# Two expert stages: the second stage's first group taken from a constant address, ahead of the tables

## The reference, cut to what matters

```python
X = fft(fft(x, axis=1), axis=2).real                 # (4, 2496, 256) -> x of 9984 rows x 256
# stage 1: each token to one expert of 8, at most 1248 tokens each
out[mask] = relu(x[mask] @ w1[e]) @ w2[e]            # w1: 256 x 1024, w2: 1024 x 256
# stage 2: each token to its best expert, no limit
e_idx = argmax(x @ w_gate)
gate_w = softmax(x @ w_gate)[e_idx];  eom = sigmoid(x @ w_output_gate)[e_idx]
out[mask] = gate_w * eom * (relu(x[mask] @ w1b[e]) @ w2b[e])
```

## Time and profile before

| | us |
|---|---|
| median of 3 runs | 1352.18 (1351.89 to 1353.84) |
| the profiled execution | 1355.83 |
| its span in the trace | 1354.1 |
| PE busy | 1277.1 (94%) |
| DVE busy | 761.8 (56%) |
| POOL busy | 520.2 (38%) |
| ACT busy | 324.8 (24%) |
| chain that ended last | PE 74%, DVE 11%, issue 2% |

### The profile page before, as it was taken

One profiled execution on the slowest core, in us unless ns is written; L12 is line 12 of the kernel. 1 busy time (PEld: TensorE's weight loads), 2 busy tenths in 40 slices (PEclk: granted clock), 3 DMA queues, 4 the chain that ended last, 5 costly groups with the idle time before them and its releaser, 6 DMA issues.

```text
span 1354.1 us, 30708 instructions
## 1 busy us (share of the span) xinstructions
PE 1277.1 (94%) x10392; PEld 1175.9 (87%) x10393; DVE 761.8 (56%) x2029; ACT 324.8 (24%) x787; POOL 520.2 (38%) x531
## 2 busy tenths in 40 slices
PE   8998999579999999999999997999999999999996
PEld 5666888558879888889999996999999999999996
DVE  6935888878585678775443544433333334333332
ACT  1013010122322323333232331222222222222221
POOL 0000011226465656555657541612443252544411
PEclk9999555579999999999999998999999999999998
DMA  7717241022212121212222221221232121232110
GB/s 322 269 62 264 91 141 64 1 76 70 83 54 87 58 83 59 75 63 87 61 84 77 68 86 43 87 68 40 78 107 74 43 90 52 77 107 75 47 39 20
DMA packets 63129, 115.98 MB, mean 86 GB/s; under 512 B 7736, under 2 KB 45377, under 8 KB 62912
## 3 DMA queue, kind: packets, MB, share of 16 engines
q1 hardware_dynamic: 39264, 72.16, 15.5%
q0 software_dynamic: 11808, 31.03, 7.0%
q10 hardware_dynamic: 11968, 11.63, 3.2%
HBM read 81.64 MB, written 34.45 MB: 86 GB/s over the span
## 4 chain that ended last, share of the span: by engine, by line
PE 74%; DVE 11%; issue 2%; DMA 1%; ACT 1%; POOL 0%; ACTq 0%; DVEq 0%; POOLq 0%; SPq 0%
PE bank L1105 22%; PE bank L1107 22%; PE bank L1106 21%; PE bank L986 3%; PE bank L969 3%; DVE hot_r L1784 2%; PE bank L1254 1%; PE bank L1117 1%; DVE hot_q L1785 1%; DVE hot_q L1783 1%; DVE hT_low L1954 1%; DVE arena L1663 1%; DVE xT_low L1947 0%; DVE arena L1728 0%; DVE arena L1657 0%
## 5 line engine op out<-in xcount | busy, mean ns | idle before, releaser
L1105 PE MATMUL bank<-weights_high,hT_high 128*128 (+1 forms) x1328 | 388.6, 293 | 0.0
L1107 PE MATMUL bank<-weights_high,hT_low 128*128 (+1 forms) x1328 | 378.4, 285 | 0.0
L1106 PE MATMUL bank<-weights_low,hT_high 128*128 (+1 forms) x1328 | 377.2, 284 | 0.0
L1105 PE MATMUL bank<-xT_high,weights_high 128*128 128x256 f32 (+2 forms) x1072 | 335.2, 313 | 9.2 <-DVE hT_low L1954 3.7
L1107 PE MATMUL bank<-xT_high,weights_low 128*128 128x256 f32 (+2 forms) x1072 | 331.1, 309 | 0.0
L1106 PE MATMUL bank<-xT_low,weights_high 128*128 128x256 f32 (+2 forms) x1072 | 330.4, 308 | 0.0
L1106 PEld LDWEIGHTS bank<-weights_low,hT_high 128*128 128x128 f32 x1328 | 250.4, 189 | 0.0
L1105 PEld LDWEIGHTS bank<-weights_high,hT_high 128*128 128x128 f32 x1328 | 250.2, 188 | 0.1
L1107 PEld LDWEIGHTS bank<-weights_high,hT_low 128*128 128x128 f32 x1328 | 250.2, 188 | 0.0
L1105 PEld LDWEIGHTS bank<-xT_high,weights_high 128*128 128x128 f32 x1072 | 204.6, 191 | 24.5 <-DVE hT_low L1954 7.8
L1107 PEld LDWEIGHTS bank<-xT_high,weights_low 128*128 128x128 f32 x1072 | 203.9, 190 | 11.3
(11 more groups left out here) (264 smaller groups left out, 1404.4 us busy)
## 6 DMA issues: line engine op xcount, KB each, us to landing
arena<-middle ACTq DMA_DIRECT2D x44, 258.0 KB
spectrum<-arena SPq DMA_DIRECT2D x39, 256.0 KB, 2.2
arena<-in_w2a_t SPq DMA_DIRECT2D x8, 1024.0 KB, 4.8
raw<-in_w1a SPq DMA_DIRECT2D x8, 1024.0 KB
raw<-in_w2a SPq DMA_DIRECT2D x8, 1024.0 KB
raw<-in_w1b SPq DMA_DIRECT2D x8, 1024.0 KB
raw<-in_w2b SPq DMA_DIRECT2D x8, 1024.0 KB
arena<-in_x SPq DMA_DIRECT2D x4, 768.0 KB, 4.4
```

The costliest lines, as they stand in the source:

```text
L1105: pe.matmul(out_, a[0], b[0], start=start, stop=False)
L1106: pe.matmul(out_, a[0], b[1], start=False, stop=False)
L1107: return pe.matmul(out_, a[1], b[0], start=False, stop=stop)
```

## The change

Expert 0 always gets at least one group (`cnt` of expert 0 is at least 1), so the first group is always rows 0 to 255 of `middle` with expert 0's weights, and needs no table. SP loads it (`first_rows`) once the last expert's first group has been scattered; `late_i` says whether expert 0 had fewer than 256 rows by then, and in that case SP waits for all scatters. TensorE turns and multiplies group 0 ahead of its wait for `m2.row`. The jump over the redo block stands ahead of group 0 on all engines; on DVE it moves ahead of `list_tables`, which follows the differences of group 0. The 24 spins go; nine stand ahead of the last `places`, and the four behind the jump follow the transposes. ACT issues the load of group 1 between the third and the fourth quarter's cast of group 0. TensorE's order for group 0 is hidden(0), read of `last_i`, result(0) tile 0, turn(1), result(0) tile 1, hidden(1); the loop starts at 1 instead of 0.

```diff
@@ SP, behind the loads of the second stage's first two weights
+            def first_rows(done):
+                sp.dma_start(xg_all, middle[0:W2, :].rearrange("(j p) r -> p j r", p=P)).then_inc(done, 16)
+
+            sp.wait_ge(m1.place, E * NG - NG + 1)
+            sp.sem_inc(s_hold, 1)
+            late = sp.value_load(late_i[0:1, 0:1], min_val=0, max_val=1)
+            sp.wait_ge(m1.sent[0], 16 * TILES[0] * E)
+            for gi in range(1, NG):
+                sp.wait_ge(m1.sent[gi], late * (16 * TILES[gi]) + 16 * TILES[gi] * (E - 1))
+            first_rows(m2.got)
             sp.wait_ge(s_flag, 1)
@@ PE, places and expert
+                    if first_count:
+                        pe.matmul(bank[7][:, w * E:w * E + E], ones_b[:], kinds_up[gi][:, :, w], start=True, stop=True)
                     pe.matmul(to, tri_b[:], ...)
...
-                        places(e, gi)
+                        elif fast:
+                            pe.wait_ge(m1.h, E * NG * FCH + 3)
+                            pe.wait_ge(m1.split, (E + 1) * SPLITS)
+                            spin(SPIN_KINDS)
+                        places(e, gi, fast and last and gi == 0)
@@ PE, behind the first stage
             list_counts()
-            pe.wait_ge(m1.h, E * NG * FCH + 3)
-            pe.wait_ge(m1.split, (E + 1) * SPLITS)
-            spin(SPIN_TABLES)
             pe.wait_ge(s_flag, 1)
...
-            spin(SPIN_BRANCH)
...
-            def result2(i):
+            def result2(i, slot=None, tiles=range(GP)):
...
+            x_turn2(0)
+            spin(SPIN_BRANCH)
+            pe.wait_ge(m2.xT, 2 * GP)
+            hidden_from(0, E % 2)
             pe.wait_ge(m2.row, 1)
             pe.sem_inc(s_hold, 1)
             last = pe.value_load(last_i[0:1, 0:1], min_val=MIN2 - 1, max_val=G2 - 1)
-            x_turn2(0)
-            hidden2(0)
-            with pe.Fori(0, last) as i:
+            result2(0, E % 2, [0])
+            x_turn2(1)
+            result2(0, E % 2, [1])
+            hidden2(1)
+            with pe.Fori(1, last) as i:
@@ ACT
-            def h_out2(i):
+            def h_out2(i, first=0, stop=HB):
...
+            x_out2(0)
+            h_out2(0, 0, HB - 1)
             for gi in range(NG):
                 act.wait_ge(m1.sent[gi], 16 * TILES[gi] * E)
+            act.wait_ge(m2.gt, GP)
             act.wait_ge(m2.row, 1)
             act.sem_inc(s_hold, 1)
+            load2(1)
             last = act.value_load(last_i[0:1, 0:1], min_val=MIN2 - 1, max_val=G2 - 1)
-            load2(0)
-            x_out2(0)
-            act.wait_ge(m2.gt, GP)
-            act.sem_inc(s_hold, 1)
-            load2(1)
-            h_out2(0)
+            h_out2(0, HB - 1)
@@ DVE
+                    if first_count:
+                        dve.tensor_scalar(late_i[:], bank[7][0:1, w * E:w * E + 1], float(W2), None, ALU.is_lt)
...
+                link(dve.tensor_scalar(cnt[:, 0:1], cnt[:, 0:1], 1.0, None, ALU.max))
...
-            list_tables(link, 1, m2.row)
             dve.wait_ge(s_flag, 1)
...
-            dve.sem_inc(m2.xT, GP)
-            dve.sem_inc(m2.h, HB)
-            dve.sem_inc(m2.y, GP)
+            x_out2(0)
+            list_tables(m2.row)
+            gate_out2(0)
+            h_out2(0)
             dve.wait_ge(m2.row, 1)
             dve.sem_inc(s_hold, 1)
             last = dve.value_load(last_i[0:1, 0:1], min_val=MIN2 - 1, max_val=G2 - 1)
-            x_out2(0)
-            h_out2(0)
             wants()
             x_out2(1)
+            gate_out2(1)
             empties()
             y_out2(0)
             h_out2(1)
```

More of the change, by code:

```diff
@@ L80 @@
 MIN2 = N // W2
-SPIN_START, SPIN_LISTS, SPIN_TURN, SPIN_TABLES, SPIN_BRANCH = 24, 12, 2, 24, 4
+SPIN_START, SPIN_LISTS, SPIN_TURN, SPIN_KINDS, SPIN_BRANCH = 24, 12, 2, 9, 4
 HB = 4
@@ L381, in build_program @@
         end_f, run_f, want_f, same_f = (sb(n, [P, G2 + 1]) for n in ("end_f", "run_f", "want_f", "same_f"))
+        late_i = sb("late_i", [1, 1], I32)
         expert_i, want_i, last_i = sb("expert_i", [1, G2], I32), sb("want_i", [1, G2 + 1], I32), sb("last_i", [1, 1], I32)
@@ L663, in _ @@
                 sp.wait_ge(again.raw, (E + 1) * 32 + 32)
+                for gi in range(NG):
+                    sp.wait_ge(again.sent[gi], 16 * TILES[gi] * E)
+                sp.wait_ge(m2.got, 16)
+                first_rows(again.raw)
+                sp.wait_ge(again.raw, (E + 1) * 32 + 48)
                 sp.sem_inc(s_hold, 1)
@@ L1153, in result, with places @@
                     mm.then_inc(m.y_ps, 1)
-                def places(e, gi):
+                def places(e, gi, first_count=False):
                     w = TILES[gi]
@@ L1206, in list_counts @@
             def list_counts():
-                pe.matmul(bank[0][:, 0:E], ones_b[:], kinds_up[NG - 1][:, :, TILES[NG - 1]], start=True,
+                pe.matmul(bank[5][:, 0:E], ones_b[:], kinds_up[NG - 1][:, :, TILES[NG - 1]], start=True,
                           stop=True).then_inc(s_list, 1)
             list_counts()
-            pe.wait_ge(m1.h, E * NG * FCH + 3)
-            pe.wait_ge(m1.split, (E + 1) * SPLITS)
-            spin(SPIN_TABLES)
             pe.wait_ge(s_flag, 1)
@@ L1244, in _ @@
                 pe.wait_ge(again.tables, 1)
+                pe.wait_ge(again.raw, (E + 1) * 32 + 48)
                 pe.sem_inc(s_hold, 1)
-            spin(SPIN_BRANCH)
             def x_turn2(i):
@@ L1267, in hidden2, with hidden_from @@
                     with pe.If(slot == s):
[L1268 to L1276, removed]
-            def result2(i):
-                slot = group_expert(i) & 1
-                for j in range(GP):
+                        hidden_from(i, s)
+            def hidden_from(i, s):
+                for q in range(HB):
+                    pe.wait_ge(m2.h, i * HB + (q + 1))
+                    for n, f in enumerate(range(q * FCH // HB, (q + 1) * FCH // HB)):
+                        for c in range(DCH):
+                            o = first_at(c, f)
+                            mm = three(bank[H_BANKS[q]][:, n * W2:(n + 1) * W2],
+                                       [t[:, o:o + P] for t in w_split[s]],
+                                       [t[:, c, 0:W2] for t in xT_split], c == 0, c == DCH - 1)
+                    mm.then_inc(m2.h_ps, 1)
+            def result2(i, slot=None, tiles=range(GP)):
+                if slot is None:
+                    slot = group_expert(i) & 1
+                for j in tiles:
                     pe.wait_ge(m2.y, i * GP + (j + 1))
@@ L1444, in x_out2 @@
                              bank[j][:, 0:D].rearrange("p (c n) -> p c n", c=DCH)).then_inc(m2.xT_high, 1)
-            def h_out2(i):
-                for q in range(HB):
+            def h_out2(i, first=0, stop=HB):
+                for q in range(first, stop):
                     act.wait_ge(m2.h_ps, i * HB + (q + 1))
@@ L1994, in routed, with placed @@
                         dve.tensor_copy(kinds_in[(gi + 1) % NG][:, :, 0], kup[:, :, w])
-                def placed(e, gi):
+                def placed(e, gi, first_count=False):
                     k0, w = FIRSTS[gi], TILES[gi]
@@ L2043, in expert @@
                             gated(e, gi)
-                        placed(e, gi)
+                        placed(e, gi, fast and last and gi == 0)
                 return x_out, h_out, expert
@@ L2051, in _ @@
             dve.sem_inc(m1.h, 3)
+            dve.sem_inc(m2.xT, GP)
+            dve.sem_inc(m2.h, HB - 1)
             name(on_limit.link, open_log)
@@ L2070, in _, with list_tables @@
             cnt_i = sb("cnt_i", [P, E], I32)
-            def list_tables(link, n, done):
-                dve.wait_ge(s_list, n)
-                link(dve.tensor_copy(quota[:], bank[0][:, 0:E]))
+            def list_tables(done):
+                dve.wait_ge(s_list, 1)
+                link(dve.tensor_copy(quota[:], bank[5][:, 0:E]))
+                dve.sem_inc(m2.h, 1)
+                dve.sem_inc(m2.y, GP)
                 link(dve.tensor_scalar(cnt_i[:], quota[:], float(W2 - 1), None, ALU.add))
@@ L2222, in _ @@
                 slow_expert(E - 1, 1, True)
-                list_tables(slow.link, 2, again.tables)
+                dve.wait_ge(s_list, 2)
+                dve.memset(same_f[:, 0:1], 0.0).then_inc(again.tables, 1)
                 dve.wait_ge(again.tables, 1)
@@ L2260, in x_out2, with gate_out2 @@
                                       hi.bitcast(F32), ALU.subtract).then_inc(m2.xT, 1)
+            def gate_out2(i):
                 for j in range(GP):
@@ L2305, in _ @@
                 x_out2(i + 1)
+                gate_out2(i + 1)
                 y_out2(i)
```

## The result

The changed kernel takes 1349.09 us (median of 15 runs, 1347.61 to 1351.15), the kernel before 1353.2 us beside it (15 runs, 1351.89 to 1355.28). The ratio is 0.9971 (95% interval 0.9964 to 0.9978): 3.9 us less, 3.0 to 4.9. It is faster, but by about half of the 7.5 us forecast, and 1349.09 lies 0.7 us above the range.

The account below looks back on a forecast made before the run. TensorE bounds the kernel; only the handover to the second group's hidden layer (846.00) can move. Hidden layer 0 starts 6.5 us earlier, takes 1.2 less, result 0 with transposes costs 0.2: 7.5 off 1352.18 gives 1344.7 us, range 1340.6 to 1348.4.

Parts of the forecast that it names:

- step 1: TensorE handover: transposes of group 0 start at 822.7, its hidden layer at 825.3; VectorE's differences end at 824.7.
- The bound: Limits of what the trace hid: TensorE's branch 1.1 to 4.9 us, next-block fetch 0 to 2.8, half clock none or throughout.
- rival C: One more instruction fetch behind the branch, on the path: 2.8 us, gain 4.7, time 1347.5; chance 0.08.
- The tables behind the differences: VectorE's tables run behind group 0's differences, 824.7 to 830.7, holding its low halves until TensorE is nearly done.
- Rival A: Branches cost only up to their start, 1.1 us each on TensorE and VectorE: gain 11.1, time 1341.1; chance 0.10.
- The clock: TensorE at half clock when the transposes start at 822.7, back at full clock 5.1 us later, at 827.8.
- Step 2: Group 0's hidden layer on TensorE: 11 matmuls at half clock (2.5 us), 37 at full (4.4), ending at 832.2.
- the sum for no half clock: With no half clock, group 0's hidden layer ends at 831.0, second group's hidden layer starts at 838.1: gain 7.9.
- steps 3 to 5: VectorE tables done 830.7, ACT's group 1 load issued 831.8, fourth low half 834.2, TensorE's second tile done 838.5.
- Rival B: TensorE's clock stays at half through group 0's hidden layer: gain 3.9, time 1348.3; chance 0.08.
- D: Expert 0 has too few rows, so SP's load waits for the last scatters, until 827.4: gain 3, 1349.2; chance 0.02.
- E: Group loop no longer stays in instruction memory; 2.8 us fetch in each of 41 passes: 107 us slower, 1459; chance 0.04.

Follow-up runs that it names:

- pad16: The changed kernel with 16 never-run instructions more in TensorE's jumped-over redo block; ratio 0.9943 to the kernel before.
- nojump_before: The kernel before without the redo block, flag read and jump on all engines; ratio 1.0007 to the kernel before.
- nojump_after: The changed kernel without the redo block, flag read and jump on all engines; ratio 0.9925 to the kernel before.
- nojump_pe: The changed kernel without the redo block, flag read and jump on TensorE alone; ratio 0.9947 to the kernel before.
- pad256: The changed kernel with 256 never-run instructions more in TensorE's jumped-over redo block; ratio 0.9967 to the kernel before.
- warm20_pad216: The changed kernel with 20 TensorE spins behind the last counts and 216 never-run instructions in the jumped-over block; ratio 0.9969 to the kernel before.
- tables_first: pad16 with the tables back ahead of VectorE's jump, as in the kernel before; ratio 0.9992 to the kernel before.
- tighter: pad16 with gate copies ahead of differences, ACT's last-group read behind its fourth cast, group 1's transposes inside result 0's second tile; ratio 0.9941 to the kernel before.

## Why the prediction was wrong

Step by step, in us behind C (the forecast's 817.71):

| step | forecast | changed | pad16 |
|---|---|---|---|
| first transpose | 5.0 | 4.9 | 4.6 |
| differences of group 0 done | 7.0 | 9.5 | 6.5 |
| hidden layer 0 starts | 7.6 | 10.2 | 7.2 |
| hidden layer 0 done, result 0 starts | 14.5 | 17.5 | 13.7 |
| tables done | 13.0 | 15.7 | 12.7 |
| load of group 1 issued | 14.1 | 17.2 | 13.8 |
| fourth low half done | 16.5 | 19.6 | 16.1 |
| second tile starts | 17.9 | 20.8 | 17.4 |
| second hidden layer starts | 20.8 | 23.7 | 20.3 |

**What failed is one term, in step 1.** The transposes were given the spacing of the kernel before, one behind the other. The bound said "another instruction block to be fetched right behind the target, 0 to 2.8 us", and I took 0, with 0.08 for the other end (rival C, 2.8 us, gain 4.7). It was the other end: 2.9 us between third and fourth transpose, gain 4.6 in the trace for 7.5 forecast. Pad16, which differs only in code that never runs and has no gap, gains 8.0. Everything behind it in the column "changed" is the forecast plus 2.5 to 3.1. The argument against C was that a fetch which runs on during short first work costs nothing. It is the other way round: short work ahead of the block's end is what does not cover it. From the return out of the jump to the first instruction of the next block it took 822.37 - 818.99 = 3.4 us, so a target with less than that much work ahead of a block's end pays at least a part of it. In pad16 about a dozen matmuls with as many weight loads run in such a stretch, some 24 of a block's 256 instructions. By this estimate about one target in ten is hit; my 0.08 was near that, but it was not counted out, and the term went into the sum as nothing for a reason that does not hold.

The trace of the kernel before could have shown it. The earlier trace rows counts three packets from 802 to 830 us, and the prediction says of them only that one must be the branch's. Asked from 824.2 us on, where TensorE comes out of its jump, to 829.4, it shows that one of them lies there:

```profile
q8 instruction: 1, 0.02, 1.3%
```

It begins 0.6 us behind the first instruction after the jump (824.78 for 824.18), as in the changed kernel (819.56 for 818.99). It cost nothing there, because TensorE had four spins to run and then waited for the load of group 0 until 829.39. The change takes that cover away too.

**What held.** The jumps as the price that the change uncovers (4.9 us on TensorE, 3.9 on VectorE, against nothing before): nojump_before and nojump_after. VectorE's jump holds the mark at 20.1 us when TensorE's is gone: nojump_pe. The tables behind the differences and what hangs on them: the column pad16 agrees with the forecast within 0.9 us at every step, and its ratio, 0.9943 of 1352.18, is 1344.5 for a forecast of 1344.7. That the two are so near is part luck: pad16's hidden layer took 1.0 us less than forecast, and the ratio's interval is 1.7 us to either side. Rival A (short jumps) fell on the 3719 ns row. The Trainium skill's rule in "Runtime: NRT & Kernel Launch", Instruction fetch mechanics, that a taken branch to a target outside the code that is held must fetch it before going on, agrees with the trace for the target's block: the branch took 3.7 us. That the block behind the target is bare as well is shown by our runs (2.8 to 3.7 us).

**The clock** was right in kind and off in size. It was at 0.50 from 3.7 to 14.0 us behind C in the changed kernel and from 4.2 to 7.7 in pad16; the forecast had it back at 10.1. The hidden layer took 7.4 and 5.9 us for a forecast of 6.9. At the mark the difference between 10.2 and 3.4 us of half clock is at most about 0.6 us (pad256 against warm20_pad216). Step 2 also misread its own row: the 5.1 us run from the first hidden matmul in the kernel before (831.76 to 836.9), but from the transposes in the forecast. From the transposes it was 7.5 us before, 9.1 in the changed kernel and 3.1 in pad16, so neither count forecasts it. And the sum for no half clock is off by 0.2: steps 3 to 5 as written give 838.3 and a gain of 7.7, not 7.9. Neither slip carries the miss. Rival B (half clock throughout) did not come; D's load was 20 us early; E's loop takes 494.8 us as before.

**The 0.7 us outside the range.** The range reached up to rival B, a gain of 3.9, and so it held rival C's 1347.5; even so the time fell outside. Its upper end stands for a gain of 1352.18 - 1348.4 = 3.8 us; measured were 3.9 by the ratio and 4.1 by the medians. As a gain, then, the result is just inside; it is outside as a time, since the kernel before gave 1353.2 in fifteen runs for 1352.18 in three; I had given the spread of the three runs (1351.89 to 1353.84) no room at the range's end.

## What to carry to other kernels

A jump over a long block costs what covers it: before work is moved ahead of tables or spins, look which sequencer events stood beside them, and price each as if bare. If the code behind the jump is on the path, look at it for a gap with "issue" in its brackets and an instruction packet in the DMA; it went with 16 or 128 instructions of padding inside the code that is jumped over, not with 4 or 256, and can come back whenever the code's length changes, so an edit of a few lines can be 3 us better or worse for no reason of its own. Compare two profiles from the last point that the edit does not move, and check that it does not, instead of by their spans.

## What the runs showed of the hardware

- The compare-and-branch over the redo block took 3.3 to 3.9 us on TensorE in the eleven profiles that have it; VectorE's first instruction stood 2.8 to 3.0 us behind the start of its branch, whose own row shows 0.07 (before, tables_first, nojump_pe).
- The end of a block right behind a jump's target cost 2.8 to 3.7 us from start to start of the two transposes around it (four profiles), and the pattern came back, to the instruction, with 256 instructions more. In pad16 the next block's packet comes just as soon behind the jump, under work, and costs nothing that the rows show.
- Spins queued ahead of a jump run on during it (817.25 to 822.2 in warm20_pad216, beside a branch of 3.3 us), and the granted clock stayed at 1.00 through it.
- Where the clock fell, it stayed at 0.50 for 3.4 us in pad16, 6.8 in tighter and 10.2 in the changed kernel, with much the same work. The hidden layer took 5.9, 7.0 and 7.4 us with it, so an estimate of this handover has a term of 1 to 1.5 us there that the runs do not fix.
